# Attention and two feed-forward layers on one core: order of the first group's attention, engines of q's copies and of the operand sums, and places of layer 1's down tiles

## The chip, the cores and the metric

The kernel runs on one core of one Trainium2 chip. Its time is the device time of one execution in microseconds (us). The core has five instruction streams that run beside one another and meet at semaphores: TensorE (PE: matmuls; PEld is its weight load), VectorE (DVE), ScalarE (ACT), GpSimd (POOL) and SyncE (SP), which here only issues DMAs. TensorE has a granted clock, shown as a share of full speed: 1.00 is its level of 2.4 GHz, 0.50 that of 1.2 GHz.

## The reference

```python
def _attn_ref(q, k, v, g_norm):          # 4 batches, 8 heads, 576 tokens, 64 per head
    kv = np.einsum('bhsd,bhse->bhde', k, v)
    out = np.einsum('bhsd,bhde->bhse', q, kv)
    rms = np.sqrt(np.mean(out * out, axis=-1, keepdims=True) + 1e-06)
    return (out / rms * g_norm)
x = attn_out.transpose(0, 2, 1, 3).reshape(2304, 512)
h = x @ w_in                             # 512 x 2048
x = (h * (1.0 / (1.0 + np.exp(-h)))) @ w_out
a = x @ w_a                              # 512 x 1536
b = x @ w_b
out = (a * b) @ w_out2
```

Everything is float32: a linear attention with a norm per head, a SiLU layer (layer 1) and a gated layer (layer 2) over 2304 tokens.

## The kernel before

**Two groups and four segments.** The tokens are worked on in two groups of 1152 (`G` 0 and 1, two batches each). The feed-forward part has four segments, `seg` 0 to 3: layer 1 of group 0, layer 1 of group 1, layer 2 of group 0, layer 2 of group 1. A segment is walked in pairs of 128 columns of d_ff: 8 pairs in segments 0 and 1, 6 in segments 2 and 3; `pp` counts all 28. `PAIR0[seg]` is a segment's first pair.

**A product in seven steps.** The product of x with a pair's weights (layer 1 has one product `u` in a pair, layer 2 two) is formed from seven block products, `STEPS`, in place of eight. Each step multiplies one sum of quarters of x (an operand, 128x1152) with one sum of quarters of the weights. Four of the seven operands are sums: n = 2 (`s1`), 1 (`s2`), 4 (`s4`) and 5 (`s3`); n = 0, 3 and 6 are quarters themselves. Each number is split into a rounded high part and a rest (`x_hi`/`x_lo`, `w_hi`/`w_lo`, `g_hi`/`g_lo`, `d_hi`/`d_lo`), and TensorE adds three products for each: a step is 12 matmuls of 288 columns. For an operand this takes, before the segment begins, the sum (DVE, `x_first` and the third of `temps`' four), the rounding (ACT, `x_round`) and the rest (DVE, `x_rest`; for the first segment three of them on POOL). ACT and DVE do it for the next segment inside the last pair of the running one (`next_round`, `next_rest`), DVE the last ones inside the first pair (`late_rest`). POOL prepares the weights in a ring of four steps (`ready`) and w_out's rows (`lower`).

**Inside a pair.** After steps 0 to 2 ACT copies PSUM aside (`part`), and TensorE's next step waits for that copy. DVE adds those copies to the PSUM results of steps 3, 5 and 6 (`add(u, 0)`, `add(u, 1)`, `add(u, 2)`); step 6 may begin only after `add(u, 1)`. ACT takes the sigmoid, DVE multiplies (`silu`), ACT rounds (`g_round`), DVE forms the rest (`g_rest`). The result times w_out, 16 down tiles of 6 matmuls in layer 1 (9 tiles in layer 2), is computed one pair later between the steps: `down1(pp - 1, n)`. The tiles alternate between two PSUM banks, and DVE adds each to its place in `xy` (`flush1`, `flush2`) before the bank's next turn.

**Attention.** Group 0's attention comes first, a head pair `h` at a time: `kv` (TensorE), `by_tiles` (q put in tile order, ACT), `q_turn` (transposes), `qT_keep` (DVE), `q_kv` (TensorE), `square` and `o_keep` (ACT, from PSUM), `sums` (DVE), `root` (ACT), `invert` and `normalise` (DVE), `o_turn` (transposes), `keep` (ACT, into `xy`). Group 1's attention is cut into 11 slots for each head pair, and one slot is done in each step of segment 0's pairs (`attend(at)`, slot `at % 11`; slot 7 is root, inverse and norm, slots 8 to 10 the last transposes).

**What sets the order.** There is no scheduler: every engine's instructions run in the order in which its block of the code is written. An instruction that waits holds all behind it on its engine. DMAs are issued by SP in the order written: k, v and q of head pairs 0 and 1, then 2 and 3, then the first weights.

The lines of the profile that come up later: L512 a step's matmuls, L559 to L561 a down tile of layer 1, L469 `q_kv`, L479 `o_turn`, L673 `by_tiles`, L899 `invert`, L734 `x_round`, L747 `part`, L906 `normalise`, L932, L934, L936 the three sums of `x_first`, L940 `x_rest`, L946 the fourth sum, L970 `add`, L979 `silu`, L1005 `g_rest`, L1019 `flush1`, L395 POOL's `x_rest`, L405 `lower`.

## Time and profile before

| what | value |
|---|---|
| median of 3 runs | 961.45 us (960.83 to 962.66) |
| the profiled execution | 962.95 us, its span 960.5 us |
| PE busy | 886.7 us (92%) |
| DVE, ACT, POOL busy | 546.0, 288.4, 590.7 us |
| mean granted clock of TensorE | 0.966 |
| DMA in the first 24 us | 206 GB/s; k, v or q of a head pair and batch 288 KB each, a load of weights 512 KB |
| share of the chain that ended last | PE 75%, DVE 13%, ACT 5% |

Busy time of an engine counts its instructions alone. The chain is followed back from the last instruction, at each step to what released it. The times in the rows are microseconds from the span's start.

### The profile page before, as it was taken

How to read it: one execution, taken by the hardware profiler on the slowest of the kernel's cores; microseconds unless marked ns; L12 is line 12 of the kernel's file. 1: busy time of each engine (PE TensorE's matmuls, PEld its weight loads, DVE VectorE, ACT ScalarE, POOL GpSimd, SP SyncE). 2: the span in 40 equal slices, each digit the busy share in tenths (PEclk: the TensorE clock that was granted, in tenths of full speed). 3: DMA queues.
4: the chain of work that ended last, by engine and by line, in shares of the span. 5: the costliest groups of instructions: out<-in, count | busy, mean ns of one | idle time of the engine just before them, and what ended most of it. 6: DMA issues, size and time to landing. Idle time of an engine off the chain costs nothing.

```text
span 960.5 us, 16917 instructions
## 1 busy us (share of the span) xinstructions
PE 886.7 (92%) x6552; PEld 837.4 (87%) x6552; DVE 546.0 (57%) x869; ACT 288.4 (30%) x459; POOL 590.7 (61%) x843
## 2 busy tenths in 40 slices
PE   4766999989898999999998999999997999999998
PEld 3666988989888999999988999999996999999996
DVE  3465555664577765555577535535658545535536
ACT  3654343343344222222243112122223112122211
POOL 0285553455356656665565758768777868768760
PEclk9768899999898999999998999999999999999999
DMA  9904140311010111111110102102111142102104
GB/s 206 210 1 118 45 117 25 96 45 44 24 45 23 45 45 46 44 45 45 44 45 23 44 23 67 45 24 65 45 45 33 56 121 67 44 25 64 45 23 98
DMA packets 38764, 55.59 MB, mean 58 GB/s; under 512 B 2592, under 2 KB 23072, under 8 KB 38688
## 3 DMA queue, kind: packets, MB, share of 16 engines
q1 hardware_dynamic: 38688, 54.54, 21.2%
q8 instruction: 53, 0.87, 0.4%
q14 instruction: 23, 0.19, 0.1%
HBM read 49.81 MB, written 4.72 MB: 57 GB/s over the span
## 4 chain that ended last, share of the span: by engine, by line
PE 75%; DVE 13%; ACT 5%; issue 4%; POOL 1%; DMA 1%; SPq 0%; ACTq 0%; DVEq 0%
PE ps L512 41%; PE ps L559 6%; PE ps L561 5%; PE ps L560 5%; PE ps L581 5%; PE ps L583 5%; PE ps L582 5%; DVE g_lo L1005 2%; PE ps L469 2%; ACT g_hi L771 2%; DVE xy L1019 2%; DVE ps L970 1%; DVE held L970 1%; PE ps L479 1%; DVE ps L979 1%
## 5 line engine op out<-in xcount | busy, mean ns | idle before, releaser
L512 PE MATMUL ps<-x_hi,w_hi 128*128 128x288 f32 x1120 | 249.1, 305 | 26.9 <-DVE held L970 17.8
L512 PE MATMUL ps<-x_lo,w_hi 128*128 128x288 f32 x1120 | 244.2, 300 | 0.0
L512 PE MATMUL ps<-x_hi,w_lo 128*128 128x288 f32 x1120 | 242.9, 299 | 0.0
L512 PEld LDWEIGHTS ps<-x_hi,w_hi 128*128 128x128 f32 x1120 | 187.0, 192 | 43.5 <-issue 19.8
L512 PEld LDWEIGHTS ps<-x_hi,w_lo 128*128 128x128 f32 x1120 | 184.7, 193 | 0.0
L512 PEld LDWEIGHTS ps<-x_lo,w_hi 128*128 128x128 f32 x1120 | 183.5, 192 | 0.0
L559 PE MATMUL ps<-g_hi,d_hi 128*128 128x288 f32 x512 | 155.1, 303 | 12.2 <-DVE xy L1019 10.8
L361 POOL TENSOR_SCALAR w_hi<-wt 128x256 fp32r<-128x256 f32 x160 | 77.3, 483 | 141.1 <-PE ps L512 136.8
L747 ACT COPY kept<-ps 128x576 f32<-128x576 f32 x120 | 77.1, 642 | 276.2 <-PE ps L512 275.6
L1019 DVE TENSOR_TENSOR xy<-xy,ps 128x288 f32<-128x288 f32 x224 | 99.1, 451 | 98.2 <-PE ps L561 96.9
L560 PE MATMUL ps<-g_lo,d_hi 128*128 128x288 f32 x512 | 153.0, 299 | 0.0
L561 PE MATMUL ps<-g_hi,d_lo 128*128 128x288 f32 x512 | 152.8, 298 | 0.0
L361 POOL TENSOR_SCALAR w_hi<-raw 128x256 fp32r<-128x256 f32 x120 | 55.3, 461 | 137.3 <-PE ps L512 137.3
L363 POOL TENSOR_TENSOR w_lo<-wt,w_hi 128x256 fp32r<-128x256 f32 x160 | 125.3, 783 | 13.3
L1029 DVE TENSOR_TENSOR xy<-xy,ps 128x512 f32<-128x512 f32 x90 | 61.6, 686 | 91.7 <-PE ps L583 91.6
L559 PEld LDWEIGHTS ps<-g_hi,d_hi 128*128 128x128 f32 x512 | 98.8, 193 | 16.2 <-issue 16.1
L363 POOL TENSOR_TENSOR w_lo<-raw,w_hi 128x256 fp32r<-128x256 f32 x120 | 96.7, 806 | 10.0
L560 PEld LDWEIGHTS ps<-g_lo,d_hi 128*128 128x128 f32 x512 | 98.3, 192 | 0.0
L561 PEld LDWEIGHTS ps<-g_hi,d_lo 128*128 128x128 f32 x512 | 98.2, 192 | 0.0
L771 ACT CAST g_hi<-ps 128x576 fp32r<-128x576 f32 x84 | 53.9, 642 | 112.3 <-DVE ps L979 57.7
L581 PE MATMUL ps<-d_hi,g_hi 128*128 128x512 f32 x216 | 85.4, 396 | 0.0
L583 PE MATMUL ps<-d_hi,g_lo 128*128 128x512 f32 x216 | 84.7, 392 | 0.0
(68 smaller groups left out, 1143.9 us busy)
## 6 DMA issues: line engine op xcount, KB each, us to landing
raw<-in_moe_w_out_dram SPq DMA_DIRECT2D x28, 512.0 KB, 3.8
raw<-in_moe_w_in_dram SPq DMA_DIRECT2D x16, 512.0 KB, 3.6
raw<-in_moe_w_a_dram SPq DMA_DIRECT2D x12, 512.0 KB, 3.6
raw<-in_moe_w_b_dram SPq DMA_DIRECT2D x12, 512.0 KB, 3.5
kvq<-in_k_dram SPq DMA_DIRECT2D x16, 288.0 KB, 6.8
kvq<-in_v_dram SPq DMA_DIRECT2D x16, 288.0 KB, 8.5
kvq<-in_q_dram SPq DMA_DIRECT2D x16, 288.0 KB, 9.8
out_dram<-xy SPq DMA_DIRECT2D x36, 128.0 KB, 2.4
```

The lines of the kernel that those rows point to most:

```text
L361: nc.gpsimd.tensor_scalar(w_hi[:, n % RING], src, 1.0, 0.0, ALU.mult, ALU.add).then_inc(w_high, 1)
L363: nc.gpsimd.tensor_tensor(w_lo[:, n % RING], src, w_hi[:, n % RING].bitcast(F32), ALU.subtract).then_inc(w_ready, 1)
L512: mm = pe.matmul(ps[:, bank + s, 0:PART], w, x[:, n, c, s * PART:(s + 1) * PART], start=(begins and first), stop=last, skip_group_check=no ...
L559: pe.matmul(dst, hi, g_hi[:, f, part], start=(f == 0), stop=False)
L560: pe.matmul(dst, hi, g_lo[:, f, part], start=False, stop=False)
L561: mm = pe.matmul(dst, lo, g_hi[:, f, part], start=False, stop=(f == 1))
L581: pe.matmul(dst, hi, d_hi[:, pp % 2, f, :], start=(f == 0), stop=False)
L583: mm = pe.matmul(dst, lo, d_hi[:, pp % 2, f, :], start=False, stop=(f == 1))
L747: nc.scalar.copy(halves(kept[:, n, :]), both(BANK_A)).then_inc(part_kept, 1)
L771: nc.scalar.copy(halves(g_at_half(g_hi, pp, m, f)), src).then_inc(g_high, 1)
L1019: nc.vector.tensor_tensor(dst, dst, src, ALU.add).then_inc(flushed, 1)
L1029: nc.vector.tensor_tensor(dst, dst, src, ALU.add).then_inc(flushed, 1)
```

## The change

1. **First group's attention.** `by_tiles` moves from ACT to POOL. `o_keep` goes: `normalise` reads `q_kv`'s result in PSUM and writes `o_sb`. TensorE does `o_turn` of a head pair right after the next one's `kv`, ahead of its `q_turn`; DVE finishes a head pair's norm before it turns to the next one's copies. SP loads the first weights (`raw` 0) ahead of head pairs 2 and 3, and POOL prepares the first four steps' weights before its share of the operands (`meanwhile`).
2. **Group 1's attention** has 12 slots: root at slot 7, inverse and norm at slot 8, last transposes at 9 to 11.
3. **Layer 1's tiles** stand 2, 3, 3, 2, 2, 2, 2 after the seven steps, in place of two after each and two more at the end. DVE's `flush` calls move to match, and `add(u, 1)` comes ahead of `g_rest(pp, 1)` and of the next segment's rests. In the first pair of layer 2 they are spread as well.
4. **Operands of segments 2 and 3**: all four sums on POOL, one in each of four pairs of the segment before. For segment 1 three stay on DVE (`x_first(1)`), the fourth goes to POOL. The rests of operands 3 and 6 of segments 1 to 3 go to POOL, operand 3's behind `lower` of the segment's last pair, operand 6's in the next segment's first pair.

```diff
+    TILES_AFTER = (2, 3, 3, 2, 2, 2, 2)
-    SLOTS = 11
+    SLOTS = 12
+    POOL_RESTS = ((0, 5, 3), (3, 6))
+    DVE_RESTS = ((1, 2, 4, 6), (0, 1, 2, 4, 5))
...
             load_heads(0, 1)
...
+            load_raw(0)
             load_heads(0, 2)
             load_heads(0, 3)
-            load_raw(0)
...
                 ready(u, 3, b21)
+                meanwhile(u)
                 ready(u, 4, b22)
...
+            def meanwhile(u):
+                pp = pair_of(u)
+                seg = seg_of(pp)
+                if u != prods_of(pp)[0]:
+                    return
+                if pp == 0:
+                    for j in range(JS):
+                        by_tiles(0, 2, j)
+                    pool.wait_ge(x_kept, UNITS // 2)
+                    pool.wait_ge(qT_mm, JS * 3)
+                    x_sum_of(0, 5)
+                    x_rest(0, 0)
+                    for j in range(JS):
+                        by_tiles(0, 3, j)
+                    x_rest(0, 5)
+                    x_rest(0, 3)
+                elif pp == PAIR0[seg]:
+                    x_rest(seg, 6)
+                elif pp == PAIR0[1] - 1:
+                    pool.wait_ge(x_kept, 2 * UNITS)
+                    x_sum_of(1, 5)
+                elif 0 < seg < len(SEGS) - 1 and pp >= PAIR0[seg] + 2 and pp < PAIR0[seg] + 6:
+                    n = (2, 1, 4, 5)[pp - PAIR0[seg] - 2]
...
+                    x_sum_of(seg + 1, n)
...
                 lower(pp)
+                if pp + 1 in PAIR0[1:-1]:
+                    x_rest(seg_of(pp) + 1, 3)
...
@@ TensorE, layer1
-                        down1(pp - 1, 2 * n)
-                        down1(pp - 1, 2 * n + 1)
-                if pp:
-                    down1(pp - 1, 14)
-                    down1(pp - 1, 15)
+                        for _ in range(TILES_AFTER[n]):
+                            down1(pp - 1, t)
+                            t += 1
@@ ScalarE, first group
                     square(0, h, j, 3 + j)
-                    o_keep(0, h, j, 3 + j)
-                if h + 1 < PAIRS:
-                    for j in range(JS):
-                        by_tiles(0, h + 1, j)
                 root(0, h)
@@ VectorE, normalise
+                    src = ps[:, 3 + j, 0:TILE3].rearrange("p (n e) -> p n e", e=HD)
...
@@ VectorE, layer1
                 silu(pp, 1)
-                flush(9)
+                flush(11)
                 attend(at + 5)
+                add(u, 1, halves(held[:, 2, :]))
                 g_rest(pp, 1)
-                next_rest(pp, 2)
-                add(u, 1, halves(held[:, 2, :]))
-                flush(10)
-                flush(11)
+                flush(12)
                 silu(pp, 2)
                 attend(at + 6)
+                flush(13)
+                next_rest(pp, 2)
+                add(u, 2, both(BANK_C))
+                flush(14)
                 g_rest(pp, 2)
-                next_rest(pp, 3)
-                add(u, 2, both(BANK_C))
-                flush(12)
-                flush(13)
+                flush(15)
                 silu(pp, 3)
-                flush(14)
-                flush(15)
                 g_rest(pp, 3)
-                next_first(pp)
+                if pp == PAIR0[1] - 2:
+                    x_first(1)
```

TensorE's rows between the first two head pairs of group 0, before; kvq_65 to kvq_68 are the buffers of head pairs 0 to 3, the lines `q_kv`, `kv`, `q_turn`, `o_turn` and `q_kv` again:

```order
L469 MATMUL ps<-kv_sb,qT_sb 64x128 x18
L444 MATMUL ps<-kvq_66 64x64 x36
L457 MATMUL ps<-ident,kvq_66 128x128 x9
L479 MATMUL ps<-ident,o_sb 128x128 x9
L469 MATMUL ps<-kv_sb,qT_sb 64x128 x18
```

And the same place in the changed kernel, in which these lines are L529, L504, L517 and L539:

```order
L529 MATMUL ps<-kv_sb,qT_sb 64x128 x18
L504 MATMUL ps<-kvq_66 64x64 x36
L539 MATMUL ps<-ident,o_sb 128x128 x9
L517 MATMUL ps<-ident,kvq_66 128x128 x9
L529 MATMUL ps<-kv_sb,qT_sb 64x128 x18
```

The transposes of the normed output have moved ahead of the next head pair's q transposes.

GpSimd's rows at the start, before; L415 is the fourth sum, L395 a rest, L374 to L363 weights, and kvq_67 holds the sum:

```order
L415 TENSOR_TENSOR kvq_67<-xy 128x1152
L395 TENSOR_TENSOR x_lo<-xy,x_hi 128x1152
L395 TENSOR_TENSOR x_lo<-kvq_67,x_hi 128x1152
L374 TENSOR_TENSOR wt<-raw 128x256
L361 TENSOR_SCALAR w_hi<-raw 128x256
L363 TENSOR_TENSOR w_lo<-raw,w_hi 128x256
L377 TENSOR_TENSOR wt<-raw,wt 128x256
L361 TENSOR_SCALAR w_hi<-wt 128x256
L363 TENSOR_TENSOR w_lo<-wt,w_hi 128x256
L395 TENSOR_TENSOR x_lo<-xy,x_hi 128x1152
```

In the changed kernel, from the weights of the fourth step on; L411 is `by_tiles`, L420 the sum, L424 a rest, L373 and L375 weights:

```order
L373 TENSOR_SCALAR w_hi<-raw 128x256
L375 TENSOR_TENSOR w_lo<-raw,w_hi 128x256
L411 COPY kvq_67<-kvq_67 128x384 x3
L420 TENSOR_TENSOR kvq_67<-xy 128x1152
L424 TENSOR_TENSOR x_lo<-xy,x_hi 128x1152
L411 COPY kvq_68<-kvq_68 128x384 x3
L424 TENSOR_TENSOR x_lo<-kvq_67,x_hi 128x1152
L424 TENSOR_TENSOR x_lo<-xy,x_hi 128x1152
L373 TENSOR_SCALAR w_hi<-raw 128x256
L375 TENSOR_TENSOR w_lo<-raw,w_hi 128x256
```

Four steps' weights now stand ahead of the sum and the rests, and q's copies between them.

VectorE's rows in segment 0's last pair, before, from the rest of the first result tile (L1005) on:

```order
L1005 TENSOR_TENSOR g_lo<-ps,g_hi 128x576
L979 TENSOR_TENSOR ps<-held,ps 128x2x288
L1019 TENSOR_TENSOR xy<-xy,ps 128x288
L1005 TENSOR_TENSOR g_lo<-ps,g_hi 128x576
L940 TENSOR_TENSOR x_lo<-kvq_65,x_hi 128x1152
L946 TENSOR_TENSOR kvq_65<-xy 128x1152
L970 TENSOR_TENSOR held<-kept,ps 128x576
L1019 TENSOR_TENSOR xy<-xy,ps 128x288 x2
L979 TENSOR_TENSOR held<-held 128x576
L1005 TENSOR_TENSOR g_lo<-held,g_hi 128x576
L940 TENSOR_TENSOR x_lo<-xy,x_hi 128x1152
L970 TENSOR_TENSOR ps<-kept,ps 128x2x288
```

In the changed kernel, where L994 is `x_rest`, L1015 `add`, L1024 `silu`, L1050 `g_rest` and L1064 `flush1`:

```order
L1024 TENSOR_TENSOR ps<-held,ps 128x2x288
L1064 TENSOR_TENSOR xy<-xy,ps 128x288
L1015 TENSOR_TENSOR held<-kept,ps 128x576
L1050 TENSOR_TENSOR g_lo<-ps,g_hi 128x576
L1064 TENSOR_TENSOR xy<-xy,ps 128x288
L1024 TENSOR_TENSOR held<-held 128x576
L1064 TENSOR_TENSOR xy<-xy,ps 128x288
L994 TENSOR_TENSOR x_lo<-kvq_65,x_hi 128x1152
L1015 TENSOR_TENSOR ps<-kept,ps 128x2x288
L1064 TENSOR_TENSOR xy<-xy,ps 128x288
L1050 TENSOR_TENSOR g_lo<-held,g_hi 128x576
L1064 TENSOR_TENSOR xy<-xy,ps 128x288
```

`add(u, 1)` (into `held`) has moved ahead of the rest of operand 2; that rest now stands right ahead of `add(u, 2)`, and the fourth sum and the rest of operand 3 are gone from the engine.

## Rows read from the trace of the kernel before

**Rows 1.** The page: busy time of TensorE, and the group of flushes.

```profile
PE 886.7 (92%) x6552; PEld 837.4 (87%) x6552; DVE 546.0 (57%) x869; ACT 288.4 (30%) x459; POOL 590.7 (61%) x843
...
L1019 DVE TENSOR_TENSOR xy<-xy,ps 128x288 f32<-128x288 f32 x224 | 99.1, 451 | 98.2 <-PE ps L561 96.9
```

**Rows 2.** TensorE's waits: who for whom, us in total, times, longest.

```profile
PE ps L512 <- DVE held L970: 17.8, 5, 4.5
PE ps L559 <- DVE xy L1019: 10.8, 14, 1.4
...
PE ps L479 <- DVE xy L1019: 4.1, 2, 2.3
...
PE ps L512 <- ACT kept L747: 2.9, 2, 2.0
PE ps L479 <- DVE xy L1017: 2.8, 1, 2.8
```

**Rows 3.** Two stretches: length, five engines' busy time, clock (0.50), DMA, GB/s.

```profile
299.65:306.48 6.83, 5.79 (x24) 5.82 (x25) 5.44 (x9) 2.95 (x4) 2.76 (x3) 0.50 0.00 0
...
729.73:733.14 3.41, 3.41 (x15) 3.22 (x14) 2.71 (x4) 1.74 (x2) 3.22 (x6) 0.50 0.00 0
```

**Rows 4.** First group's last two head pairs: start, us, instruction, idle before, releaser.

```profile
36.15 2.19 PE L469 MATMUL ps<-kv_sb,qT_sb 128*64 128x128 f32 x36
...
41.02 1.35 ACT L673 COPY kvq<-kvq 128x384 f32<-128x384 f32 x3
...
43.62 0.26 DVE L899 RECIPROCAL stat<-stat 128x18 f32<-128x18 f32 x1
...
46.63 4.05 PE L469 MATMUL ps<-kv_sb,qT_sb 128*64 128x128 f32 x36
...
52.48 2.53 DVE L906 TENSOR_TENSOR o_sb<-o_sb,stat 128x384 f32<-128x384 f32 x3
...
56.64 0.85 PE L512 MATMUL ps<-x_hi,w_hi 128*128 128x288 f32 x2 [0.67 <-ACT xy L699]
```

**Rows 5.** GpSimd and VectorE side by side at the first steps.

```profile
57.85 2.65 POOL L395 TENSOR_TENSOR x_lo<-xy,x_hi 128x1152 fp32r<-128x1152 f32 x1 [2.25 <-ACT x_hi L734]
...
58.01 3.71 DVE L934 TENSOR_TENSOR kvq<-kvq,xy 128x1152 f32<-128x1152 f32 x1
```

**Rows 6.** End of pair 6 and start of pair 7 (segment 0's last), in time order.

```profile
273.67 0.75 DVE L970 TENSOR_TENSOR ps<-kept,ps 128x576 f32<-128x576 f32 x1
...
274.92 0.37 PE L559 MATMUL ps<-g_hi,d_hi 128*128 128x288 f32 x1 [0.69 <-DVE xy L1019]
...
277.82 1.35 DVE L932 TENSOR_TENSOR kvq<-xy 128x1152 f32<-128x1152 f32 x1
278.37 0.64 ACT L747 COPY kept<-ps 128x576 f32<-128x576 f32 x1 [1.80 <-PE ps L512]
...
280.68 1.78 DVE L936 TENSOR_TENSOR kvq<-xy,kvq 128x1152 f32<-128x1152 f32 x1
...
282.97 0.37 PE L559 MATMUL ps<-g_hi,d_hi 128*128 128x288 f32 x1 [1.44 <-DVE xy L1019]
```

**Rows 7.** From segment 1 to segment 2, in time order.

```profile
504.72 1.61 DVE L940 TENSOR_TENSOR x_lo<-kvq,x_hi 128x1152 fp32r<-128x1152 f32 x1
...
506.37 1.43 DVE L946 TENSOR_TENSOR kvq<-xy 128x1152 f32<-128x1152 f32 x1
...
508.61 0.82 PE L512 MATMUL ps<-x_hi,w_hi 128*128 128x288 f32 x2 [3.11 <-DVE held L970]
...
516.45 1.16 ACT L734 CAST x_hi<-xy 128x1152 fp32r<-128x1152 f32 x1
```

**Rows 8.** Slot 7 of group 1's last head pair, in pair 5.

```profile
240.10 1.50 DVE L906 TENSOR_TENSOR o_sb<-o_sb,stat 128x384 f32<-128x384 f32 x3 [0.16 <-DVE stat L899]
...
243.07 0.82 PE L512 MATMUL ps<-x_hi,w_hi 128*128 128x288 f32 x2 [3.58 <-DVE held L970]
```

**Rows 9.** GpSimd with one input, two instructions of 512 elements.

```profile
227.73 1.22 POOL L405 TENSOR_SCALAR d_hi<-raw 128x512 fp32r<-128x512 f32 x2
```

More of the change, by code:

```diff
@@ L231, in fused_attention_ffn_kernel @@
                 turns += SLOT_BANKS[at % SLOTS] if at < SLOTS * PAIRS else 0
-                for _ in range(2 if pp else 0):
+                for _ in range(TILES_AFTER[n] if pp else 0):
                     tile_turn.append(turns)
                     turns += 1
-            for _ in range(tiles - (2 * steps if pp else 0)):
+            for _ in range(tiles if steps == 0 else 0):
                 tile_turn.append(turns)
@@ new lines, in x_sum_of, with x_rest @@
+            def x_sum_of(seg, n):
+                G = SEGS[seg][0]
+                s1, s2, s4, s3 = temps(seg)
+                a11, a12, a21, a22 = quad(G, 0, 0), quad(G, 0, 1), quad(G, 1, 0), quad(G, 1, 1)
+                dst, a, b, op = {2: (s1, a21, a22, ALU.add), 1: (s2, s1, a11, ALU.subtract),
+                                 4: (s4, a12, s2, ALU.subtract), 5: (s3, a11, a21, ALU.subtract)}[n]
+                nc.gpsimd.tensor_tensor(dst, a, b, op).then_inc(side_sum, 1)
+            def x_rest(seg, n):
+                pool.wait_ge(x_high, x_rounded(seg, n))
+                nc.gpsimd.tensor_tensor(x_lo[:, n], operand(seg, n), x_hi[:, n].bitcast(F32),
+                                        ALU.subtract).then_inc(side_ready, 1)
@@ L410, in lower @@
                                             ALU.subtract).then_inc(d_ready, 1)
-            pool.wait_ge(x_kept, UNITS // 2)
-            pool.wait_ge(qT_mm, JS * 3)
-            nc.gpsimd.tensor_tensor(operand(0, 5), quad(0, 0, 0), quad(0, 1, 0), ALU.subtract).then_inc(side_sum, 1)
-            x_rest(0)
-            x_rest(5)
+            for h in range(2):
+                for j in range(JS):
+                    by_tiles(0, h, j)
             for pp in range(PAIR0[-1]):
@@ L646, in _ @@
                     kv(0, h + 1)
+                for j in range(JS):
+                    o_turn(0, h, j, j)
+                if h + 1 < PAIRS:
                     for j in range(JS):
                         q_turn(0, h + 1, j, j)
-                for j in range(JS):
-                    o_turn(0, h, j, j)
             pe.wait_ge(x_kept, UNITS)
@@ L842, in _ @@
             act.wait_ge(consts, 3)
-            for j in range(JS):
-                by_tiles(0, 0, j)
             for h in range(PAIRS):
@@ L847, in _ @@
                     square(0, h, j, 3 + j)
-                    o_keep(0, h, j, 3 + j)
-                if h + 1 < PAIRS:
-                    for j in range(JS):
-                        by_tiles(0, h + 1, j)
                 root(0, h)
@@ L1044, in layer1 @@
                 flush(3)
+                flush(4)
                 late_rest(pp, 1)
@@ L1047, in layer1 @@
                 attend(at + 2)
-                flush(4)
                 flush(5)
+                flush(6)
+                flush(7)
                 late_rest(pp, 2)
@@ L1077, in layer1, with flush @@
-                flush(13)
+                flush(15)
                 silu(pp, 3)
-                flush(14)
-                flush(15)
                 g_rest(pp, 3)
-                next_first(pp)
+                if pp == PAIR0[1] - 2:
+                    x_first(1)
             def layer2_after_1(pp):
                 ua, ub = prods_of(pp)
-                flush1(pp - 1, 0)
+                def flush(first, last):
+                    for n in range(first, last + 1):
+                        flush1(pp - 1, n)
@@ L1151, in layer2 @@
                 g_rest(pp, 3)
[L1152 removed]
+            kv_keep(0, 0)
+            for j in range(JS):
+                qT_keep(0, 0, j, j)
             for h in range(PAIRS):
[L1155 to L1161 removed]
                 for j in range(JS):
                     sums(0, h, j)
[L1164 to L1166 removed]
+                invert(0, h)
+                for j in range(JS):
+                    normalise(0, h, j)
+                if h + 1 < PAIRS:
+                    kv_keep(0, h + 1)
+                    for j in range(JS):
+                        qT_keep(0, h + 1, j, j)
             x_first(0)
```

173 lines of the change are left out of this document (80 added, 93 removed).

## The prediction

> **What bounds the kernel now.** I read the page first, then TensorE's waits, then the clock by stretches, then the timeline around each long wait. TensorE is busy 886.7 of 960.5 us [rows 1], so only time in which it stands still or runs at the lower clock can be won. The waits [rows 2] name few places. Five waits, 17.8 us together, are step matmuls waiting for `add`: once in pair 0, once at slot 7 of group 1's last head pair [rows 8], and once at each of the three changes of segment, the longest, 4.5, at the last ([rows 7] show the middle one). Down tiles wait 10.8 us in 14 waits for flushes, group 1's transposes 4.1 + 2.8 us for flushes, steps 2.9 us for `part`. The second loss is the clock: after each of the five waits for `add` it falls. The stretch after one of them is 6.83 us long at 0.50 [rows 3], so it costs half of that, 3.4 us; the one at the change to segment 3 is 3.41 long and costs 1.7. Before 56.64 us, where the first step begins, TensorE is paced by attention's own chain [rows 4].
>
> **Why the waits for `add` are there.** At a change DVE runs a rest of 1.61 and the fourth sum of 1.43 before `add(u, 1)`, and step 6 begins 3.11 late [rows 7]. At slot 7 it is `normalise`, 1.50, behind a root for which DVE waits: 3.58 [rows 8].
>
> **The change part by part**, as gains (+) of time.
>
> *A, first group: +4.5.* The last two head pairs' `q_kv` begin 10.5 apart, and the first step comes 10.0 after the last [rows 4]. Between them root stands behind q's copies on ACT (1.35 for three), and the inverse, 7.5 after `q_kv` (43.62), behind the next head pair's copies on DVE. In the new order nothing but root stands before it. The copies begin 4.9 after `q_kv`; with root alone in their place the inverse begins at about 5.5, 2.0 earlier, and up to 0.6 more since the rounding of operand 0 no longer falls among the squares. Given back is 0.9: q's transposes are now behind the norm. I take 1.7 for this head pair and, at the lower clock, 1.0 for the one before. Behind the last one the norm takes 1.5 in place of 2.53, and ACT is 0.8 freer: 1.8. Head pair 0 gains nothing: its copies start earlier, but the table load in front of them now stands in front of the first square. The first weights push head pairs 2 and 3 back by 0.5 MB at 206 GB/s, 2.5 us (the table), still ahead of their use. Bounds: 0 (if the loads or the clock pace all of it) and 8 (full clock throughout). A copy of q on GpSimd has no row: by 1.22 for two of 512 elements [rows 9] it is 0.46, by the two-input rate, 2.65 for 1152 [rows 5], 0.9. I take 0.5, since it has one input; only the first of three delays a transpose.
>
> *B, pairs 0 and 1: +5.0.* `add(u, 1)` is ahead of one `g_rest` (0.7); `add(u, 2)` too, so `part` comes 1.0 earlier; the wait of 2.8 before the first `o_turn` becomes about 1.1, because the norm now delays one flush instead of a transpose; the lower clock after it (3.4) I count half, 1.7. Bounds 1 and 8.
>
> *C, group 1's attention: +12.3.* Gone: 3.58 + 3.4 [rows 3, 8], 4.1 of transposes [rows 2], 2.6 of flush waits. Root is done a step ahead of the inverse. Added: in pair 2 the norm falls on step 6 behind ACT's two table loads and delays a flush, 1.4.
>
> *D, three sums of segment 1's operands: -4.6.* They stay on DVE. They run 277.82 to 282.4, and a tile waits 1.44, after 0.69 before [rows 6]. Call E the end of step 6. A step or two tiles take 1.65: (282.97 - 1.44 - 274.92)/4. Before, two tiles more stood behind E. Now TensorE asks for the flush at E + 4 x 1.65 = 6.6. DVE: `add` 0.75, flush 0.45, rest 0.75, flush 0.45, `silu` 0.75, ACT's round 0.65, rest 0.75: E + 4.6; sums 4.6, flush 0.45: E + 9.6, plus up to 0.8 if GpSimd gets in between. Wait 3.0 to 3.8; I take 3.3, and since waits of 3.1 and more were each followed by the lower clock, 3.4 more. 2.1 - 6.7 = -4.6; without the clock -1.2.
>
> *E, G and J, the changes of segment.* `add(u, 1)` is no longer behind anything: 3.1 + 3.4, 3.1 + 3.4, and 4.5 + 0.9 + 1.7 go, 20.1 [rows 2, 3, 7]. What is late next: `x_rest` of operand 2 (1.35, up to 1.61) now stands before `add(u, 2)`, of which 1.1 is late, and ACT rounds operand 6 (1.16 [rows 7]) before `part`. In an ordinary pair `part` ends at E + 0.75 + 0.45 + 0.75 + 0.45 + 0.75 + 0.65 + 0.65 = 4.45, and TensorE wants it at E + 3 x 1.65 = 4.95, 0.5 to spare. At a change it ends at 4.45 + 1.1 + 1.16 = 6.7: a wait of 1.75 into segment 1; into segment 2, where one tile stands after the first step, TensorE is there at 4.1 and waits 2.6; into segment 3, with longer tiles, 1.5. For the 2.6 I count half a clock fall, 1.7. Gains 4.8, 2.2 and 5.5: +12.5.
>
> *F, ordinary pairs of layer 1: +6.9.* Four tiles in a row waited 0.69 for a flush behind `add(u, 2)`. With at most three tiles together and the flush next in line DVE keeps up: seven waits of 0.69, one of 0.74 in the first pair of layer 2, and the 1.44 before segment 2, whose sums go to GpSimd.
>
> *GpSimd's new work* is 12 instructions of 2.65 and hides behind the ring of four steps: a sum stands behind the fourth step's weights at a pair's start, the fifth step's are wanted over 8 us later. Rest 6 waits for ACT's round at E + 6.5 and holds weights 4 until E + 11; step 4 comes after E + 15 in layer 1, some 2 us later than needed in segment 3. Uncovered it would cost those 2.65.
>
> Sum: 4.5 + 5.0 + 12.3 - 4.6 + 12.5 + 6.9 = 36.6. The profiled execution took 962.95, so 926.3; it stands 1.5 over the median, so 925.
>
> **The port, a rule against this change.** A sum on DVE took 3.71 while GpSimd's instruction of 2.65 ran, against 1.35 for its like [rows 5, 6]: it waited until GpSimd was through. The Trainium skill, "SBUF — State Buffer", section "Who interferes with whom", says that the port pair which both share is locked for a whole instruction, and that a DVE instruction with two SBUF inputs needs it, one with at most one does not. The trace agrees; by it `normalise` from PSUM is free of GpSimd. The first rival rests on such a collision.
>
> **Rivals.**
> 1. *GpSimd's sums take the port first.* In four pairs of segment 1 the sum is issued at E + 0.1 + 0.4 + 0.75 = 1.3, and `g_rest` of the result tile in `held` (both inputs in SBUF) at E + 0.75 + 0.45 = 1.2. DVE asks a tenth earlier, so I expect it to win. If not, it waits 2.65, `part` ends at 7.1, TensorE waits 2.2: four times, 8.8. Time 934.
> 2. *The changes of segment refill.* If `x_rest` and ACT's queue are 1 to 1.5 us later than reckoned, each wait is 3 or more and the clock falls as before: all 12.5 of it stays. Time 938. For it: ACT has no slack there. Against: the reckoning takes every duration from rows.
> 3. *The waits stay short of a clock fall*, at D and into segment 2, and the first group runs at full clock: 3.4 + 1.7 + 3.5 more. Time 916.
> 4. *The first group does not follow its order* but the clock, as in A's lower bound: 930.
> 5. *Slower.* Each of 15 pair boundaries of layer 1 now has only 0.5 to spare before `part`, where four tiles used to cover it. If DVE or ACT lag there in every pair by d, the loss is 15 x (d - 0.5). It passes the whole gain from d = 2.9; at waits of 3.0 each the time is 925 + 45 = 970. Against: the chain's engines are half idle in these pairs, DVE 57% and ACT 30% busy [rows 1].
>
> **How the numbers follow.** Forecast (925, own range 918 to 932) 0.50; rivals 1 to 5: 0.15, 0.13, 0.09, 0.08, 0.05. Rivals 3 (916) and 2 (938) bound four fifths; with A's and D's unknown costs (3 to 4 each way) the range is 908 to 943. Shorter or longer by under 0.2% (1.9 us) could not be told from no change: faster 0.94, same 0.02, slower 0.04.
>
> **What would show it.** The first step at 52 (right) or 56 (A wrong). No wait of a step for `add` after pair 0. A wait for a flush of 3 to 4 us at about 265, followed by clock 0.50. At the changes, waits for `part` of 1.5 to 2.6. No wait per pair at down tiles. PE's busy time about 870. Wrong: `g_rest` of over 2 us beside a sum on GpSimd (rival 1), or a wait for `part` in every pair (rival 5).

## The result, and the profile after

The changed kernel takes 930.67 us (median of 4 runs, 930.59 to 931.23) against 961.32: the ratio is 0.968, 95% interval 0.9664 to 0.9697. The forecast was 925.0. The profiled execution took 930.64 us, 32.3 less than before's 962.95; the forecast had 36.6. Its span is 928.4. The page of the changed kernel answers [rows 1] so:

```profile
PE 875.0 (94%) x6552; PEld 829.5 (89%) x6552; DVE 530.0 (57%) x854; ACT 276.5 (30%) x435; POOL 624.7 (67%) x870
```

TensorE is 11.7 us less busy with the same 6552 matmuls, in part because fewer of them run at the lower clock. TensorE's waits in the changed kernel answer [rows 2]; L572 is a step, L615 a down tile, L539 `o_turn`, L803 `part`, L1015 `add`, L1064 the adding flush, L375 the low halves of the weights on GpSimd:

```profile
PE ps L539 <- DVE o_sb L963: 11.0, 4, 3.4
...
PE ps L615 <- DVE xy L1064: 6.8, 4, 3.1
PE ps L572 <- ACT kept L803: 6.6, 5, 2.8
PE ps L572 <- POOL w_lo L375: 3.6, 2, 2.3
...
PE ps L572 <- DVE held L1015: 2.9, 1, 2.9
```

Steps wait for `add` once in place of five times, down tiles for a flush four times in place of fourteen. Waits for `part` rose from 2.9 to 6.6 us, and GpSimd, for which steps waited 0.2 us in all before, now holds them up for 3.6. No transpose of group 1 waits over 1.3 us any more, where the longest took 2.8.

The clock, with [rows 3] to compare: five of the stretches of the changed kernel at 0.50, and one ordinary pair of layer 1 (columns as there):

```profile
51.44:65.09 13.65, 9.80 (x101) 8.97 (x102) 11.15 (x11) 8.19 (x12) 6.97 (x6) 0.50 0.00 1
140.19:147.02 6.83, 6.11 (x26) 6.12 (x27) 4.16 (x8) 2.51 (x4) 0.63 (x2) 0.50 0.00 0
266.48:269.89 3.41, 3.41 (x16) 3.41 (x16) 0.91 (x2) 0.00 (x0) 1.03 (x2) 0.50 0.33 97
293.79:297.20 3.41, 3.41 (x17) 3.41 (x16) 2.35 (x2) 0.64 (x1) 3.26 (x4) 0.50 0.00 0
488.35:491.76 3.41, 3.13 (x13) 3.16 (x14) 0.96 (x1) 0.14 (x1) 3.41 (x1) 0.50 0.00 0
314.82:338.92 24.10, 24.10 (x183) 24.00 (x182) 14.58 (x28) 6.97 (x12) 14.53 (x23) 1.00 0.14 46
```

In all 37.5 us of the changed kernel's span are at 0.50, against 64.8 before. The last row shows a pair in which TensorE never stops: 24.10 us, all of them busy.

Where the time came from is read best by landmarks, the start of the first matmul of a pair's first step in the two traces (pairs counted from 0; the forecast's terms belong to the stretch that ends there):

```
start of                       before    after   gained in stretch   forecast
pair 0 (first step)             56.64    52.05        4.6            A 4.5
pair 2                         122.94   110.11        8.2            B 5.0
pair 7 (segment 0's last)      276.59   258.19        5.6            C 12.3, a wait of D's 0.7: 13.0
pair 9                         333.42   314.82        0.2            rest of D, a wait of F's, into segment 1: 0.2
pair 21 (segment 2's last)     693.12   663.93       10.6            rest of F, into segment 2: 8.4
pair 27 (the last)             909.40   877.26        2.9            into segment 3: 5.5
end (profiled time)            962.95   930.64        0.2            0
```

Two waits of 0.69 in the kernel before lie one stretch ahead of the rest of their term: that of D at 274.92 and the first of F's seven at 331.75. So B and F were underrated by 3.2 and 2.2, C's stretch and the last change of segment overrated by 7.4 and 2.6.

**The first group** [rows 4]. In the changed kernel's timeline (start, us, instruction, idle before and who ended it) the last two `q_kv` (L529) begin 9.3 apart, not 10.5. The inverse (L949) of the first of these two head pairs stands 4.7 behind its `q_kv`, not 7.5, and the last head pair's norm (L963) takes 1.49, not 2.53:

```profile
34.66 2.19 PE L529 MATMUL ps<-kv_sb,qT_sb 128*64 128x128 f32 x36
...
39.37 0.27 DVE L949 RECIPROCAL stat<-stat 128x18 f32<-128x18 f32 x1 [0.38 <-ACT stat L750]
...
43.96 2.48 PE L529 MATMUL ps<-kv_sb,qT_sb 128*64 128x128 f32 x36
...
49.28 1.49 DVE L963 TENSOR_TENSOR o_sb<-ps,stat 128x384 f32<-128x384 f32 x3
...
52.05 0.85 PE L572 MATMUL ps<-x_hi,w_hi 128*128 128x288 f32 x2 [0.68 <-ACT xy L759]
```

**Pair 2** is where most of C went. The timeline of VectorE, ScalarE and TensorE there, in the order of time:

```profile
133.97 1.28 ACT L750 ACT_TABLE_LOAD   x1
...
135.59 1.28 ACT L814 ACT_TABLE_LOAD   x1
136.88 0.69 ACT L814 ACTIVATE held<-held 128x576 f32<-128x576 f32 x1
...
137.60 0.86 DVE L1024 TENSOR_TENSOR held<-held 128x576 f32<-128x576 f32 x1 [1.61 <-ACT held L814]
...
138.68 1.73 DVE L963 TENSOR_TENSOR o_sb<-o_sb,stat 128x384 f32<-128x384 f32 x3
140.33 0.44 DVE L1064 TENSOR_TENSOR xy<-xy,ps 128x288 f32<-128x288 f32 x1
...
140.91 0.58 PE L615 MATMUL ps<-g_hi,d_hi 128*128 128x288 f32 x1 [2.76 <-DVE xy L1064]
```

`silu` (L1024) waits for a sigmoid behind two table loads; the flush that TensorE needs is queued behind `silu` and the norm. TensorE stands 2.76 us, and then comes the stretch of 6.83 at 0.50.

**The change to segment 1** [rows 6]. First the three sums that stayed on VectorE (L986 to L990), then ScalarE's rounding of operand 6 ahead of `part`:

```profile
261.13 1.35 DVE L986 TENSOR_TENSOR kvq<-xy 128x1152 f32<-128x1152 f32 x1
...
265.67 0.81 DVE L1064 TENSOR_TENSOR xy<-xy,ps 128x288 f32<-128x288 f32 x2
...
266.26 0.39 PE L615 MATMUL ps<-g_hi,d_hi 128*128 128x288 f32 x1 [3.11 <-DVE xy L1064]
...
290.58 1.16 ACT L790 CAST x_hi<-xy 128x1152 fp32r<-128x1152 f32 x1
291.63 0.64 ACT L803 COPY kept<-ps 128x576 f32<-128x576 f32 x1
...
292.42 0.50 PE L572 MATMUL ps<-x_hi,w_hi 128*128 128x288 f32 x2 [1.89 <-ACT kept L803]
```

**The change to segment 3.** GpSimd's timeline: the rest of operand 3 (L424, 2.68) stands ahead of the first step's weights, and the step waits for their low half; the rest of operand 6 stands ahead of a later step's, and that step waits too:

```profile
694.40 2.68 POOL L424 TENSOR_TENSOR x_lo<-xy,x_hi 128x1152 fp32r<-128x1152 f32 x1
...
699.92 1.10 POOL L375 TENSOR_TENSOR w_lo<-raw,w_hi 128x256 fp32r<-128x256 f32 x1
...
701.08 0.53 PE L572 MATMUL ps<-x_hi,w_hi 128*128 128x288 f32 x2 [2.26 <-POOL w_lo L375]
...
707.05 2.67 POOL L424 TENSOR_TENSOR x_lo<-xy,x_hi 128x1152 fp32r<-128x1152 f32 x1
...
712.06 0.53 PE L572 MATMUL ps<-x_hi,w_hi 128*128 128x288 f32 x2 [1.35 <-POOL w_lo L375]
```

**The port** that VectorE and GpSimd share (first rival). In each of the four pairs of segment 1 with a sum on GpSimd, VectorE's `g_rest` of the tile in `held` starts just ahead of it, and takes its usual 0.75. The first of them:

```profile
338.69 0.75 DVE L1050 TENSOR_TENSOR g_lo<-held,g_hi 128x576 fp32r<-128x576 f32 x1
...
338.76 3.20 POOL L420 TENSOR_TENSOR kvq<-xy 128x1152 f32<-128x1152 f32 x1
```

### The profile page after: what moved, and what is told of

It reads as the page before. It is cut to its first block, busy times and chain, and to the rows that moved or that the text cites. A ratio compares the mean times of both kernels' runs of the same rounds, so it can differ in the third digit from the quotient of the medians.

```text
span 928.4 us, 16906 instructions
## 1 busy us (share of the span) xinstructions
PE 875.0 (94%) x6552; PEld 829.5 (89%) x6552; DVE 530.0 (57%) x854; ACT 276.5 (30%) x435; POOL 624.7 (67%) x870
## 4 chain that ended last, share of the span: by engine, by line
PE 84%; DVE 7%; ACT 3%; POOL 2%; issue 2%; DMA 1%; SPq 0%; ACTq 0%; DVEq 0%; POOLq 0%
PE ps L572 44%; PE ps L615 7%; PE ps L616 7%; PE ps L617 7%; PE ps L637 5%; PE ps L639 5%; PE ps L638 5%; PE ps L529 1%; PE ps L517 1%; PE ps L539 1%; DVE g_lo L1050 1%; ACT sq L738 1%; DMA kvq<-in_q_dram 1%; POOL w_lo L375 1%; DVE xy L1064 1%
## 5 line engine op out<-in xcount | busy, mean ns | idle before, releaser
L572 PE MATMUL ps<-x_hi,w_hi 128*128 128x288 f32 x1120 | 245.9, 301 | 17.6 <-ACT kept L803 6.6
L572 PE MATMUL ps<-x_lo,w_hi 128*128 128x288 f32 x1120 | 242.2, 298 | 0.0
L572 PE MATMUL ps<-x_hi,w_lo 128*128 128x288 f32 x1120 | 241.3, 297 | 0.0
L572 PEld LDWEIGHTS ps<-x_hi,w_hi 128*128 128x128 f32 x1120 | 185.4, 190 | 31.9 <-issue 18.4
L572 PEld LDWEIGHTS ps<-x_hi,w_lo 128*128 128x128 f32 x1120 | 182.9, 191 | 0.0
L572 PEld LDWEIGHTS ps<-x_lo,w_hi 128*128 128x128 f32 x1120 | 181.4, 190 | 0.0
L373 POOL TENSOR_SCALAR w_hi<-wt 128x256 fp32r<-128x256 f32 x160 | 74.1, 463 | 144.2 <-PE ps L572 140.0
L615 PE MATMUL ps<-g_hi,d_hi 128*128 128x288 f32 x512 | 156.2, 305 | 9.5 <-DVE xy L1064 6.8
L803 ACT COPY kept<-ps 128x576 f32<-128x576 f32 x120 | 77.1, 643 | 264.2 <-PE ps L572 263.8
L1064 DVE TENSOR_TENSOR xy<-xy,ps 128x288 f32<-128x288 f32 x224 | 100.7, 451 | 82.3 <-PE ps L617 81.3
L375 POOL TENSOR_TENSOR w_lo<-wt,w_hi 128x256 fp32r<-128x256 f32 x160 | 123.5, 772 | 13.3
L615 PEld LDWEIGHTS ps<-g_hi,d_hi 128*128 128x128 f32 x512 | 98.6, 193 | 13.2 <-issue 10.8
L373 POOL TENSOR_SCALAR w_hi<-raw 128x256 fp32r<-128x256 f32 x120 | 54.7, 456 | 76.7 <-PE ps L572 76.6
L375 POOL TENSOR_TENSOR w_lo<-raw,w_hi 128x256 fp32r<-128x256 f32 x120 | 92.1, 767 | 10.0
```

The costliest lines, as they stand in the source:

```text
L373: nc.gpsimd.tensor_scalar(w_hi[:, n % RING], src, 1.0, 0.0, ALU.mult, ALU.add).then_inc(w_high, 1)
L375: nc.gpsimd.tensor_tensor(w_lo[:, n % RING], src, w_hi[:, n % RING].bitcast(F32), ALU.subtract).then_inc(w_ready, 1)
L572: mm = pe.matmul(ps[:, bank + s, 0:PART], w, x[:, n, c, s * PART:(s + 1) * PART], start=(begins and first), stop=last, skip_group_check=no ...
L615: pe.matmul(dst, hi, g_hi[:, f, part], start=(f == 0), stop=False)
L803: nc.scalar.copy(halves(kept[:, n, :]), both(BANK_A)).then_inc(part_kept, 1)
L1064: nc.vector.tensor_tensor(dst, dst, src, ALU.add).then_inc(flushed, 1)
```

## The experiments

Twelve kernels ran, in three batches, and each batch had the kernel before in it: its medians there are 961.93 (part 1, `add(u, 1)` first, tiles, 11 slots), 961.26 (port, `flush(13)`, segment 1's sums, operand 6) and 961.57 (the other four). Ratios are to it, with their 95% interval. Diffs are cut, `...` marks what is left out.

### Parts of the change alone, put into the kernel before

**Part 1** (first group's order, q's copies on GpSimd, norm from PSUM), nothing else:

```diff
@@ TensorE, first group
                 if h + 1 < PAIRS:
                     kv(0, h + 1)
+                for j in range(JS):
+                    o_turn(0, h, j, j)
+                if h + 1 < PAIRS:
                     for j in range(JS):
                         q_turn(0, h + 1, j, j)
-                for j in range(JS):
-                    o_turn(0, h, j, j)
...
@@ GpSimd
+                nc.gpsimd.tensor_copy(dst, src).then_inc(q_ready, 1)
```

> The kernel before with part 1 alone: q's copies on GpSimd, norm from PSUM, new order of the first group, first weights loaded and prepared earlier. In the changed kernel the first step comes at 52.05 us, 4.6 earlier. Theory: that is this part's own doing and it carries through, so 961.3 - 4.6 = 956.7, first step near 52. Rival: the first group is paced by its loads or by the lower clock, and the 4.6 are given back by pair 0 or by a later fall of the clock: 959 to 961.

Measured 958.41, ratio 0.9961 (0.9945 to 0.9976). The first step begins at 53.55, 3.1 earlier. The theory holds in direction; the time lies nearer the rival's. What follows is nearly unchanged, as TensorE's waits show (L529 a step, L576 a down tile):

```profile
PE ps L529 <- DVE held L990: 17.8, 6, 4.5
PE ps L576 <- DVE xy L1039: 12.6, 17, 1.4
```

**`add(u, 1)` first**, alone:

```diff
                 attend(at + 5)
+                add(u, 1, halves(held[:, 2, :]))
                 g_rest(pp, 1)
                 next_rest(pp, 2)
-                add(u, 1, halves(held[:, 2, :]))
...
                 g_rest(pp, 1)
+                add(ub, 1, halves(held[:, 4, :]))
                 next_rest(pp, 2)
-                add(ub, 1, halves(held[:, 4, :]))
```

> The kernel before with one move alone: add(u, 1) ahead of the rests and the fourth sum, nothing else. Rival (the change is only about the wait for add): the three waits for add at the changes of segment go with their clock falls, some 20 us less the waits for part of 1.5 to 2.6: about 948. Theory: the 3 us of operand work then stand ahead of the flushes and of add(u, 2), so the waits move to the down tiles (1.8 and 2.8 us at each change in layer 1) and to part (some 4 us into segment 3), and the clock falls all the same: 958 to 963, no wait for add of over 1 us at a change of segment.

Measured 962.9 (959.6 to 964.3 in ten times), ratio 1.0004 (0.9991 to 1.0017): nothing. The waits, of the profiled execution, which with 959.6 is the shortest of the ten, tell why:

```profile
PE ps L559 <- DVE xy L1019: 21.7, 18, 3.3
...
PE ps L512 <- ACT kept L747: 7.3, 3, 4.5
PE ps L512 <- DVE held L970: 6.8, 3, 2.9
```

Against [rows 2], waits for `add` fell by 11.0 us, those of tiles for flushes rose by 10.9, those for `part` by 4.4. The wait only changed its name and place.

**Tiles spread over the steps**, alone:

```diff
+    TILES_AFTER = (2, 3, 3, 2, 2, 2, 2)
...
-                        down1(pp - 1, 2 * n)
-                        down1(pp - 1, 2 * n + 1)
+                        for _ in range(TILES_AFTER[n]):
+                            down1(pp - 1, t)
+                            t += 1
...
-                g_rest(pp, 2)
+                flush(13)
                 next_rest(pp, 3)
                 add(u, 2, both(BANK_C))
-                flush(12)
-                flush(13)
+                flush(14)
+                g_rest(pp, 2)
+                flush(15)
                 silu(pp, 3)
```

VectorE's flushes move with the tiles. One more thing moves with them: `g_rest(pp, 2)` now stands behind `add(u, 2)`, which belongs to the forecast's B.

> The kernel before with layer 1's tiles at 2, 3, 3, 2, 2, 2, 2 and the flushes moved to match, nothing else. Theory: the waits of 0.69 at four tiles in a row go in all pairs of layer 1 (some 8 us), the waits for add at the changes stay, and the two waits behind the three sums grow from 2.1 to 3.3 as they did in the changed kernel (3.1), each with a fall of the clock of 1.7: 961.3 - 8.3 + 2.4 + 3.4 = 959; 956 if only one of them takes the clock down. Rival: spreading is pure gain, 953.

Measured 959.07, ratio 0.9972 (0.9955 to 0.9989), as expected:

```profile
PE ps L513 <- DVE held L969: 17.3, 5, 4.5
PE ps L560 <- DVE xy L1018: 10.1, 6, 3.0
```

The waits of 0.69 are gone (6 waits in place of 14), but fewer, longer ones of up to 3.0 took their place; those for `add` stayed.

**The three together**:

> The kernel before with three parts of the change at once: the first group's new order with q's copies on GpSimd and the norm from PSUM, the tiles spread over the steps, and add(u, 1) ahead of g_rest and next_rest. Attention keeps 11 slots, all later operand sums stay on VectorE. One at a time they gave 2.9, 2.3 and -1.5 us. Theory A (the parts cover for each other: taken alone, a wait for add turns into one for a flush, or the other way, and both go only together): the seven waits of 0.69 and most of those for add at the three changes go, 961.3 - 2.9 - 6 - 3 to 5 = 948.5 (946 to 951). Theory B (the parts add up, and the rest of the change's gain lies in the 12th slot and in GpSimd's sums alone): 961.3 - 3.7 = 957.6 (956 to 959).

Measured 954.78, ratio 0.9929 (0.9914 to 0.9944): 6.8 us. The single gains in that expectation were reckoned against 961.3; against the kernel before in their own batch they are 3.5, 2.9 and -1.0, 5.4 in all, and with intervals of over 1 us either way on each, 6.8 can't be told from their sum. The time lies outside both ranges, 3.8 above A's and 1.2 below B's. Theory A falls; that the three parts add up, as B has it, agrees with the times, and half of B's miss is that reckoning.

```profile
PE ps L577 <- DVE xy L1038: 13.1, 8, 3.0
...
PE ps L530 <- ACT kept L766: 10.8, 5, 4.5
PE ps L530 <- DVE held L989: 6.3, 3, 2.9
```

The waits for `add` at the three changes are down to one of 1.0, but `part` (10.8 us, against 2.9 in [rows 2]) and the flushes there are late in their place, since VectorE still does all the sums and rests.

### Parts taken back out of the changed kernel

**11 slots for attention** in place of 12:

```diff
-    SLOTS = 12
-    SLOT_BANKS = (2, 1, 1, 1, 1, 1, 1, 0, 0, 1, 1, 1)
+    SLOTS = 11
+    SLOT_BANKS = (2, 1, 1, 1, 1, 1, 1, 0, 1, 1, 1)
```

> The changed kernel with 11 slots again, root, inverse and norm in one slot (part 2 undone). Prediction's step C: the 12th slot frees 3.58 and a clock fall of 3.4 in pair 5 and costs 1.4 in pair 2, so without it 930.7 + 5.6 = 936. Theory after seeing the trace (in pair 2 the norm behind two table loads costs 2.76 and a clock fall of 3.4): the slot takes away one such wait and makes another, so 930 to 933 without it, with a wait of about 3 for add in pair 5 and none of 2.76 for a flush in pair 2.

Measured 943.84, ratio 0.9813 (0.9799 to 0.9828). The twelfth slot, a second one that is empty for TensorE, is worth 13.2 us, more than either theory had. By the landmarks 1.3 of it is the first step's start (53.37 and 52.05), which the slots do not touch, 3.7 lie in pairs 0 and 1, 7.3 in pairs 2 to 6 and 1.3 at the change to segment 2, where the clock fell for 6.83 and not 3.41. With eleven, in the head pairs' turns TensorE waits 2.79 us at 86.27, 2.48 at 138.04, 3.05 at 186.04 and 2.45 at 237.91, and a stretch at 0.50 follows each (6.83, then 3.41 three times); with twelve it waits 1.15, 2.76 and 1.28 there, and one stretch of 6.83 follows the 2.76. Up to the last matmul it is 61.4 us at 0.50 against 37.5, which is worth up to 12.0. Two rows of its waits that are 0 and 1.3 in the changed kernel:

```profile
PE ps L539 <- DVE xy L1062: 2.8, 1, 2.8
PE ps L539 <- DVE xy L1064: 2.5, 1, 2.5
```

With the kernel of three parts this gives a ledger: 961.3 before, 954.8 with the three parts, 943.8 with GpSimd's sums and rests, VectorE's new order at the changes and the spread tiles of layer 2's first pair (11.0), 930.7 with the twelfth slot (13.1).

**The sums of segments 2 and 3 back on VectorE**:

```diff
-            if n == 5 or seg >= 2:
+            if n == 5:
...
-                if pp == PAIR0[1] - 2:
-                    x_first(1)
+                next_first(pp)
```

> The changed kernel with the three sums of the operands of segments 2 and 3 back on VectorE, at the end of the last pair but one of the segment before, as in the kernel before; the fourth sum and all the rests stay where the change put them. Theory: into segment 2 it is the same as the three sums that had stayed in segment 1, which cost a wait of 3.1 us for a flush and 1.7 of clock: 4.8; into segment 3 a tile of the second layer takes twice as long and leaves VectorE room: 0 to 1.5. So 930.7 + 5.5 = 936.2 (934.5 to 938.5). Rival: GpSimd's sums cost as much as they save (its weights are late by 2.3 and 1.4 us at the change to segment 3), so 930 to 932.

Measured 934.10, ratio 0.9713 (0.9693 to 0.9734): 3.4 more, just under the theory's range. The wait is there, 2.71 us for a flush at 461.95, with 3.41 us at 0.50 behind it (1.7). GpSimd's weights are still late by 2.27 and 1.38 us at the change to segment 3, so its sums aren't what makes them late. The profiled execution, 931.86, is the shortest of the four (up to 936.05), and in it the clock does not fall at the change to segment 2, behind a wait of 2.79; so the trace accounts for 1.2 of the 3.4.

**VectorE asks for the port later**:

```diff
                 flush(14)
-                g_rest(pp, 2)
                 flush(15)
+                g_rest(pp, 2)
```

> The changed kernel, with flush(15) ahead of g_rest(pp, 2) on VectorE in ordinary layer 1 pairs. In segment 1's pairs GpSimd's weight sum (3.2 us) then asks for the shared port before VectorE's g_rest, where in the changed kernel VectorE asks 0.07 us sooner (338.69 against 338.76). Theory (the rival of the forecast, 'the sums take the port first'): g_rest(2) is held up to 2.6 us in each of four pairs, the down tiles of the next pair that read it wait about 2.2 us each: 930.7 + 8.8 = 939.5 (934 to 941). Other side: the tiles that read it start late enough, or VectorE gets the port all the same; 930 to 932.

Measured 944.68, ratio 0.9827 (0.9811 to 0.9843): 14.0 more than the changed kernel, for one flush of 0.45 us moved. In its timeline GpSimd's sum now starts 0.73 ahead of `g_rest`, which takes 2.56 in place of 0.75; `part` (L803) follows late, and TensorE waits 1.81:

```profile
341.54 2.67 POOL L420 TENSOR_TENSOR kvq<-xy 128x1152 f32<-128x1152 f32 x1
...
342.27 2.56 DVE L1050 TENSOR_TENSOR g_lo<-held,g_hi 128x576 fp32r<-128x576 f32 x1
...
346.06 0.65 ACT L803 COPY kept<-ps 128x576 f32<-128x576 f32 x1
...
346.86 0.50 PE L572 MATMUL ps<-x_hi,w_hi 128*128 128x288 f32 x2 [1.81 <-ACT kept L803]
```

The wait of 1.81 comes five times, in the four pairs and in pair 7 (9.1 us); 10.3 us more are at 0.50 than in the changed kernel (up to 5.1), though not all of them where the port is lost. The stretch from pair 9 to pair 16, which has the four pairs, takes 180.4 us in place of 168.5, and 1.3 of the 14.0 lie before the first step, which the edit does not touch. The first rival's mechanism is real. It had four waits of 2.2, 8.8; the runs show four of 1.81, two falls of the clock of 3.41 us among them, and a fifth wait in pair 7: 11.9 in the four pairs' stretch alone.

### Repairs of what the forecast had too cheap

**`flush(13)` ahead of `silu(pp, 2)`**:

```diff
                 flush(12)
+                flush(13)
                 silu(pp, 2)
                 attend(at + 6)
-                flush(13)
```

> The changed kernel, with flush(13) (two copies of down tile 13 out of PSUM, VectorE) put ahead of silu(pp, 2) and attend(at + 6) in every ordinary layer 1 pair. In the changed kernel TensorE stands 2.76 us in pair 2 (138.16) for that copy, which is queued on VectorE behind silu(2), and silu(2) waits there for a sigmoid that ScalarE runs late; behind the stall the clock is at .5 for 6.83 us, which costs 3.4. Theory: the wait is one of queue order alone, so both go, and tile 14 or the turn of the next slot waits up to 1.5 us instead: 930.7 - 4.7 = 926.0 (925 to 928). Rival: VectorE's work of pair 2 is late as a whole, the copy only stands first in the line; then the wait reappears at tile 14 or at the first tile of pair 3 with its fall of the clock: 930 to 931.

Measured 924.96, ratio 0.9617 (0.96 to 0.9633), 5.7 less than the changed kernel. In pair 2 TensorE now waits 1.84 at 140.18, a transpose of the slot for a flush, and the stretch behind it is 3.41 and not 6.83 long; pair 2 itself takes 28.7 us in place of 32.4. Of the other 2.0, 1.7 is that the clock does not fall at the change to segment 2, though the wait there is 2.60. Waits for adding flushes are down from 6.8 to:

```profile
PE ps L615 <- DVE xy L1064: 3.5, 2, 3.1
```

The price of pair 2 was in good part the order of one queue, as the theory has it.

**Segment 1's sums on GpSimd too** (in pair 7):

```diff
-            if n == 5 or seg >= 2:
+            if n == 5 or seg >= 1:
...
-                if pp == PAIR0[1] - 2:
-                    x_first(1)
```

> The changed kernel, with the three Strassen sums of segment 1 that had stayed on VectorE (about 1.2 us each, in pair 6) done by GpSimd in pair 7 like those of segments 2 and 3. Theory: VectorE's queue in pair 6 is what the 3.11 us wait at 263.15 and the clock of .5 for 3.41 us behind it come from (1.7 more), so 930.7 - 4.8 = 925.9 (925 to 927.5). Rival: GpSimd has no room for 3 x 3.2 us ahead of pair 8's operands, the weights' low halves or the operands come late at the change of segment (290.5), and 2 to 5 us come back there: 928 to 931.

Measured 927.41, ratio 0.9645 (0.963 to 0.966): 3.3 less, inside the theory's range. The 3.11 us wait is gone, and the rival is half right: a step (L575 here) waits 3.78 for the weights where `part` had held it 1.89:

```profile
PE ps L575 <- POOL w_lo L375: 6.0, 2, 3.8
```

**Operand 6 rounded behind `part(u, 0)`**:

```diff
                 g_round(pp, 3)
-                next_round(pp, 6)
...
                 part(u, 0)
+                last_round(pp)
```

> The changed kernel, with ScalarE's rounding of operand 6 of the next segment (1.15 us) moved behind the first add of that segment's first pair, part(u, 0). In the changed kernel TensorE waits for part at each change of segment: 1.89 us at 290.53, 2.76 us at 485.87, with the clock at .5 for 3.41 us behind each. Theory: ScalarE's row is what makes part late, so each wait falls by 1.15 and, at 0.75, the clock stays up behind the first at least: 930.7 - 3 x 1.0 - 1.7 to 3.4 = 925 to 926.5. Rival: part waits for its product's last matmul or for the bank rather than for ScalarE's queue, so the move changes nothing: 930 to 931; or operand 6 is late where it is read: over 931.

Measured 925.64, ratio 0.9627 (0.9612 to 0.9641): 5.0 less. Waits for `part` fall from 6.6 to 2.0 us:

```profile
PE ps L572 <- POOL w_lo L375: 4.8, 3, 2.3
...
PE ps L572 <- ACT kept L803: 2.0, 3, 1.3
```

Into segments 1 and 2 GpSimd's weights are the next in line, at 0.84 and 1.74, and the clock does not fall there; it falls for 3.41 us at the change to segment 3 instead, behind a wait of 2.27.

**Both repairs** (the first and the third):

> The changed kernel with flush(13) ahead of silu(pp, 2), and ScalarE's rounding of operand 6 behind part(u, 0), together. One at a time they gave 5.7 and 5.0 us. The first acts in pair 2, the second at the changes of segment, so they add up: 930.7 - 10.7 = 920.0 (918.5 to 922). Rival: some of each gain was the clock in the first group, which ran one stretch of 3.41 us less at half speed in both, and that counts once: 921.5 to 923.

Measured 921.78, ratio 0.9586 (0.957 to 0.9601), 8.9 less than the changed kernel, in both ranges. What counts once is the clock: at the change to segment 2 either repair alone had gained its 1.7, and over the whole span the 37.5 us at 0.50 are 30.7 with either repair and 30.7 with both.

**Both, and the rest of operand 3 of segment 3 on VectorE**:

```diff
-    POOL_RESTS = ((0, 5, 3), (3, 6))
-    DVE_RESTS = ((1, 2, 4, 6), (0, 1, 2, 4, 5))
+    POOL_RESTS = ((0, 5, 3), (3, 6), (3, 6), (6,))
+    DVE_RESTS = ((1, 2, 4, 6), (0, 1, 2, 4, 5), (0, 1, 2, 4, 5), (0, 1, 2, 3, 4, 5))
...
                 g_rest(pp, 3)
+                next_rest(pp, 3)
```

> As the kernel with both edits, and with the rest of operand 3 of segment 3 back on VectorE, behind g_rest(pp, 3). In the changed kernel and in the one with operand 6 rounded later, steps of the first pair of segment 3 wait 2.27 us for the low halves of the weights, which GpSimd makes behind that rest (2.68 us). Theory: GpSimd is then on time, ScalarE's part is on time too since its rounding stands behind it, so the 2.27 and the clock's 1.7 go: 4.0 less than the kernel with both, 916 (915 to 918). Rival: the wait passes to VectorE's x_lo or to part, 1.5 to 2.3 us, and nothing is gained: 919 to 921.

Measured 920.68, ratio 0.9568 (0.9552 to 0.9585), not told apart from the one without. The 2.3 us wait at the change is gone, and the second one, 1.60 us with both repairs alone, is 2.17. GpSimd's timeline there (L420 is a rest, L371 the low half, L568 a step):

```profile
696.92 3.79 POOL L420 TENSOR_TENSOR x_lo<-xy,x_hi 128x1152 fp32r<-128x1152 f32 x1
...
702.27 0.72 POOL L371 TENSOR_TENSOR w_lo<-raw,w_hi 128x256 fp32r<-128x256 f32 x1
...
703.05 0.53 PE L568 MATMUL ps<-x_hi,w_hi 128*128 128x288 f32 x2 [2.17 <-POOL w_lo L371]
```

It is the other rest, that of operand 6, that holds these weights. This kernel is the fastest measured, 10.0 us below the changed one.

## Why the prediction was right, and where its steps were off

**A, right in size, with a caution.** 4.6 against 4.5. But in the kernels with the new first group the first step begins anywhere from 51.7 to 53.7 us, and in the three with the old one from 55.6 to 56.6: at 52.05 in the changed one, where two stretches of 3.41 us at 0.50 lie before 51 us, at 53.55 in the one with part 1 alone, where three do and a long one begins at 49.5. So up to 1.6 us of A's agreement is chance: A lies between 2 and 5, and part 1 alone gained 3.5. Of its steps, the inverse came 4.7 behind `q_kv` where I had 5.5 or up to 0.6 less.

**B, the right mechanism, mis-sized by 3.2.** The wait ahead of the first `o_turn` became 1.15 us for a flush, as forecast (1.1), and all waits from pair 0 to pair 2 fell by 3.4 us, 12.6 to 9.2, which is what B's other terms had (3.4). What I had halved was the clock: in pairs 0 and 1, 13.0 us are at 0.50 (51.44 to 65.09), against 24.6 before, worth 5.8 where I had put 1.7.

**C, the step that missed most.** The place was named rightly (the norm on step 6 of pair 2, behind two table loads, delaying a flush) and priced at 1.4. It costs 2.76 + 3.4 = 6.2, and the kernel with `flush(13)` moved gets 3.7 back in that pair. I had counted the norm's delay, and not that `silu` itself waits for the sigmoid behind those loads with everything queued behind it. Another 2.7 us are waits of 0.76, 1.28 and 0.64 us in pairs 2, 4 and 5 that I had put at zero. Together these are 7.5, and the stretch missed by 7.4. That the twelfth slot is the largest single gain is shown by its removal, 13.2 us, though 3.7 of it are B's, 1.3 chance before the first step and 1.3 the clock at segment 2.

**D and the change to segment 1: right.** The wait for a flush is 3.11 (forecast 3.3), that for `part` 1.89 (1.75). Behind the first the clock fell for 3.41 us where I had taken 6.83, and behind the second it fell too, where I had said it would not: 1.7 less and 1.7 more. That these two cancel is luck. The kernels without the three sums on VectorE and without the early rounding confirm the two causes.

**The change to segment 2: right.** 2.76 us for `part` (forecast 2.6). The clock's fall cost 1.7, the very term in the sum, though I had come to it as an even chance of a fall twice as long.

**The change to segment 3, the wrong engine.** The forecast had 1.5 us for `part`. It is GpSimd's weights, 2.26 and 1.35, behind its two rests. The prediction had named one of them (rest 6 holds the weights some 2 us too long in segment 3) and then not put it into the sum; that is the wait of 1.35. The larger one, 2.26 behind the rest of operand 3, it had not named at all. The kernel that took operand 3's rest away shows that each rest holds the weights by itself: the first wait went and the second stayed.

**F, right, 2.2 better.** All waits per pair are gone (the terms that F lists add up to 7.0, not the 6.9 in the sum). An ordinary pair fell from 25.19 to 24.10 us, by 1.1 and not 0.69: TensorE's busy time in the pair fell by 0.3 too, from 24.40 to 24.10, with the same matmuls. A pair of segment 1 takes 24.1 in the kernel with only the tiles spread as well, so this comes with that edit; what shortens the busy time no run shows.

**The rivals.** The first did not happen by 0.07 us, and the experiment shows that it would have cost 12 to 14. The second (the waits for `part` reach 3 us, and all falls of the clock stay as before) did not happen: the waits were 1.89 and 2.76, with one stretch of 3.41 behind each where there had been 6.83, and no fall at the last change, where there had been 3.41. The third (no fall at D and into segment 2) is refuted by the stretches at 266.48 and 488.35. The fourth has a time, 930, next to the measured 930.7, and its condition still failed: the first step came at 52.05 and not at 56. What took the time up to it is mostly C. The fifth is refuted: no ordinary pair has a wait for `part`, until the port is lost; then 1.81 each.

**The terms do not belong to one edit each.** `add(u, 1)` first is the heart of E, G and J (12.5 forecast), and alone it brings nothing; the gain at the changes is there only once GpSimd has the sums and rests. The sum came out near because each term was worked out with the other edits in place, and because misses of both signs met in it: +3.2 and +2.2, -7.4 and -2.6. The second reason is luck.

## What to carry to other kernels

Price a reordering with everything else in place: a wait that one edit removes passes to the next in the queue until that is moved too, as the edit that shifted 11.0 us of waits from one name to another and gained nothing shows. When an instruction waits for another engine, count what stands behind it in its own queue before you count its own delay; one flush moved ahead of such a wait brought 5.7 us, 3.7 of them in the pair where it stood. And where two engines ask for one port within a tenth of a microsecond, look for a margin: here it was 0.07 us wide and 12 to 14 us dear.
